# Scores of k's first 128 channels ahead of the others, and another order of M's pieces, in a fused attention and two-layer kernel

## The chip, the cores and the metric

The kernel runs on one core of a Trainium2 chip. The metric is the device time of one execution in microseconds; before the change it is 1213.12 us, the median of 3 runs (1212.65 to 1213.14).

## The reference

Shapes: q, k, v are 1 x 6016 x 256, w_in is 256 x 2048, w_out 2048 x 256, w_gate and w_val 256 x 1536, the last w_out 1536 x 256, all float32.

```python
qn = q / (norm(q, axis=1) + 1e-6);  kn = k / (norm(k, axis=1) + 1e-6)
s = kn.transpose(0, 2, 1) @ qn / tau          # 256 x 256, contracted over 6016 tokens
a = exp(s - s.max(-1));  a /= a.sum(-1) + 1e-9
x = v @ a                                     # 6016 x 256
h = x @ w_in                                  # 6016 x 2048
g = (a0 + a1 h + a2 h^2 + a3 h^3) / (1 + |b0||h| + |b1| h^2 + 1e-6)
y = g @ w_out                                 # 6016 x 256
out = (sigmoid(y @ w_gate) * (y @ w_val)) @ w_out2
```

The kernel computes M = a @ w_in once (256 x 2048), so that h = v @ M.

## The kernel before, in words

Each engine has a program of its own, written out by hand; between engines there are only semaphores, and each engine works its queue in order. Nothing plans or reorders. SP's queue (and ScalarE's for the first small chunks) issues the loads.

**Scores.** k and q arrive as 47 tiles of 128 tokens in 16 chunks (sizes 1 1 1 1 2 2 3, then 4). For each tile TensorE (L840 to L847) multiplies k's channels 0 to 127 by q (c = 0) and k's channels 128 to 255 by q (c = 1), 256 columns each in full float32, which the trace shows as two records a product. The two sums stay in two PSUM banks. ScalarE squares each chunk (L421, L425), VectorE adds the squares (L620, L627). `norms()` (L820) sums them over the partitions with TensorE, at tile NORMS_AT = 42 of 47. ScalarE takes roots (L434 to L440), VectorE reciprocals (L632, L634).

**Softmax.** For c = 0 and 1 VectorE scales the scores (L637) and takes the row minimum of the negated ones (L639), ScalarE takes the exponential with its row sum (L446), TensorE turns it (L854, 2 transposes), VectorE copies it to SBUF as `att_t` (L642). TensorE runs 8 spare products (L850, no result is used) before the first turn.

**M in pieces.** `M_TILES` lists pieces (half c, columns lo to hi) of M. `m_tile` (L806) makes one with two products into one of four banks; `split_m` splits it into a high part (ScalarE, L412) and a low part (VectorE, L594), which also applies the row's 1/sum. The first M_FIRST = 4 pieces are made behind the turns; the others (`M_AT`) in slots 0 to 5 of block 0.

**Blocks.** The 6016 tokens go in 16 blocks of 376 columns. A block has 8 slots j, each with a pair of 128 channels of h: TensorE `hidden` (12 products in a three-product float32r scheme, L801 to L803), ScalarE reads h twice (in block 0 L496 and L498, later L532 and L535; the second raises `h_read`), `vb` (L506, L551), VectorE the rational function (L714, L716, `first_quad` L679, L685, L688, L695 in block 0; L745 to L777 later), TensorE adds w_out times g. In block 0 that uses the raw w_out (`add_raw_y`, L902) two slots behind. y's gate and value tiles follow a block behind, from slot 2 of block 1 on. From block 2 on a loop runs.

**Weights.** The 13 chunks of w_out, w_gate, w_val, w_out2 are staged raw, copied to a high part by ScalarE (`weights_hi`, L400) and a low part by GpSimd (`weights_lo`, L372, from two SBUF operands). A chunk's staging space is reused by a later chunk, whose load on SP's queue waits for the low part. Before: high parts 0 to 3 before the norms, 4 after them, 5 behind M's first pieces, 6 to 12 in slots 1 to 7 of block 0; low parts 0 to 4 before the blocks, 5 in slot 0, 6 to 11 in slots 2 to 7, 12 in slot 0 of block 1, each after `h_read`. TensorE waits for all low parts in slot 2 of block 1 (L952).

Of the kernel before, what the change touches and what calls it, by code (L numbers as in the profile page):

```python
# [20 lines left out]
def attention_rational_gated_kernel(nc, q, k, v, tau, w_in, w_out1, coef_a, coef_b, w_gate, w_val, w_out2, out):  # L21
# [34 lines left out]
    M_BOUNDS = [0, P, 2 * P, 4 * P] + list(range(6 * P, FF1, BANK)) + [FF1]  # L56
    M_TILES = [(c, lo, hi) for lo, hi in zip(M_BOUNDS, M_BOUNDS[1:]) for c in range(CC)]
    M_FIRST = 4
    M_LOW = sum(lo < FF1 // 2 for _, lo, _ in M_TILES)
    M_AT = ((4, 5, 6, 7), (8, 9), (10,), (11,), (12,), (13,))  # L60
    assert M_FIRST + sum(len(a) for a in M_AT) == len(M_TILES)
# [9 lines left out]
    assert sum(KQ_SIZES) == NT  # L71


    W1_CHUNKS = T1 // 4
    EARLY_HI, EARLY_LO, COEF_AFTER = 6, 5, 6
    COEF_SPREAD_BEFORE = 9
    FIRST_SPARES, SOFTMAX_SPARES, SEAM_SPARES = 5, 8, 7
    NORMS_AT = NT - 5

    with ExitStack() as ctx:  # L80
# [96 lines left out]
        ps_attt = [ps[:, 6 + c, 0:C].rearrange("p (a b) -> p a b", a=CC) for c in range(CC)]  # L177
# [7 lines left out]
        kq_multiplied, squared, summed = sem("kq_multiplied"), sem("squared"), sem("summed")  # L185
        norms_summed, norms_rooted, small_step = sem("norms_summed"), sem("norms_rooted"), sem("small_step")
# [42 lines left out]
        assert EARLY_HI + PAIRS - 1 == EARLY_LO + PAIRS == len(chunks)  # L229
# [122 lines left out]
        def _(pool):  # L352
# [26 lines left out]
            def step(i, first, carry, head, tail):  # L379
                for j, now, late, old, gone, early, second, left in slots(i, first, carry, head, tail):  # L380
                    if is_block(i, 0) and j != 1 or is_block(i, 1) and j == 0:
                        pool.wait_ge(h_read, now + 1)
                        weights_lo(EARLY_LO + max(now - 1, 0))
                    if old is not None and not unsplit(old):
                        n = j % 2
                        pool.wait_ge(g_hi_ready, old + 1)
                        wait_count(pool, y_added, old + (-1))
                        nc.gpsimd.tensor_tensor(g_lo[n], g[n], as_f32(g_hi[n]),  # L388
                                                ALU.subtract).then_inc(g_lo_ready, 1)
# [5 lines left out]
        def _(act):  # L395
# [12 lines left out]
            def split_m(n):  # L408

                c, lo, hi = M_TILES[n]  # L410
                act.wait_ge(m_done, n + 1)
                nc.scalar.activation(m_hi[:, c, lo:hi], ps[:, M_BANKS[n % len(M_BANKS)], 0:hi - lo], ACT.Identity,  # L412
                                     scale=row_inv[:, c:c + 1]).then_inc(m_hi_ready, 1)
# [16 lines left out]
            act.wait_ge(kq_multiplied, sum(2 * t * C < 2 * CC * FF1 + 2 * T1 * C for t, _ in KQ_CHUNKS))  # L430
            for n in range(W1_CHUNKS):
                weights_hi(n)
# [10 lines left out]
            weights_hi(W1_CHUNKS)  # L443
# [4 lines left out]
            act.wait_ge(exps_ready, CC)  # L448
            nc.scalar.activation(row_sum, row_sum, ACT.Identity, bias=sum_guard).then_inc(sums_guarded, 1)
            act.wait_ge(row_inv_ready, 1)  # L450
            for n in range(M_FIRST):
                split_m(n)
            weights_hi(W1_CHUNKS + 1)
# [30 lines left out]
            def first_slot(j):  # L484
# [25 lines left out]
                if j != 1:  # L510
                    first_seed(max(j - 1, 0))
                if j > 0:
                    weights_hi(EARLY_HI + j - 1)

            def step(i, first, carry, head, tail):
                if splits_v(i, first):
                    split_v(i)
                for j, now, late, old, gone, early, second, left in slots(i, first, carry, head, tail):
# [26 lines left out]
                    if is_block(i, 1) and j == 1:  # L545
                        act.wait_ge(w_lo_ready, len(chunks))
# [38 lines left out]
        def _(dve):  # L585
# [49 lines left out]
            dve.wait_ge(kq_multiplied, len(KQ_CHUNKS))  # L635
            for c in range(CC):
                link(nc.vector.scalar_tensor_tensor(out=att[:, c, :], in0=ps_kq[:, c, :], scalar=k_inv[:, c:c + 1],  # L637
                                                    in1=q_inv, op0=ALU.mult, op1=ALU.mult))
                nc.vector.tensor_reduce(neg_min[:, c:c + 1], att[:, c, :], AX_X, ALU.min).then_inc(scores_ready, 1)  # L639
            for c in range(CC):  # L640
                dve.wait_ge(att_turned, c + 1)
                nc.vector.tensor_copy(att_t[:, :, c * P:(c + 1) * P], ps_attt[c]).then_inc(att_t_ready, 1)  # L642
            dve.wait_ge(sums_guarded, 1)
            nc.vector.reciprocal(row_inv, row_sum).then_inc(row_inv_ready, 1)
            dve.wait_ge(row_inv_ready, 1)
# [151 lines left out]
        def _(pe):  # L797
# [35 lines left out]
            spare_products(FIRST_SPARES)  # L833
            for n, (t, w) in enumerate(KQ_CHUNKS):
# [5 lines left out]
                for x in range(w):  # L840
                    if t + x == NORMS_AT:
                        norms()
                    for c in range(CC):
                        last = nc.tensor.matmul(ps_kq[:, c, :], k_in[n][:, x * C + c * P:x * C + (c + 1) * P],  # L844
                                                q_in[n][:, x * C:(x + 1) * C],
                                                start=(t + x == 0), stop=(t + x == NT - 1))
                last.then_inc(kq_multiplied, 1)  # L847

            pe.wait_ge(ident_ready, 1)
            spare_products(SOFTMAX_SPARES)  # L850
            for c in range(CC):
                pe.wait_ge(exps_ready, c + 1)
                for d in range(CC):
                    last = nc.tensor.transpose(ps_attt[c][:, d, :], att_e[:, c, d * P:(d + 1) * P], ident[:])  # L854
                last.then_inc(att_turned, 1)
            for n in range(M_FIRST):
                m_tile(n)

            def hidden(i, j, pair):
# [8 lines left out]
                for x in range(2):  # L868
                    f = slice((2 * j + x) * P, (2 * j + x + 1) * P)
                    if is_block(i, 0):  # L870
                        pe.wait_ge(m_lo_ready, sum(lo < f.stop for _, lo, _ in M_TILES))
# [126 lines left out]
```

## Time and profile before

| | |
|---|---|
| median of 3 runs | 1213.12 us |
| the profiled execution | 1212.42 us |
| its span | 1210.0 us |
| TensorE busy | 1195.0 us (99%) |
| VectorE busy | 1068.1 us (88%) |
| ScalarE busy | 882.5 us (73%) |
| GpSimd busy | 250.4 us (21%) |
| granted TensorE clock | 1.00 |

The span is what the profiler saw from the first to the last instruction; the execution's own time is somewhat longer. Busy TensorE is modelled: its products are pipelined and a row's length reaches over the next one's start, so the distance between starts is what one costs. A timeline row with a count is several instructions put together, from the first one's start to the last one's end. "idle before" is what an engine stood for in front of a row, and the arrow says who released it. In the chain of waits pieces follow each other without overlap. PE is TensorE, PEld its weight loads, DVE VectorE, ACT ScalarE, POOL GpSimd; `work`, `ps` and `before` are big buffers which hold many things.

### The profile page before, as it was taken

The page shows a single profiled execution, that of the slowest core. Times are in us where ns is not written, and L with a number is a line of the kernel's source. Part 1 is how long each engine was busy: PE and PEld are TensorE (multiplying, and loading weights), DVE is VectorE, ACT ScalarE, POOL GpSimd, SP SyncE. Part 2 cuts the span into 40 slices and gives each one's busy share as a digit, 9 for nine tenths or more (in the row PEclk, how much of TensorE's full clock was granted, in tenths as well). Part 3 has the DMA queues.
Part 4 walks back from the last instruction along what each step waited for, and adds up shares of the span by engine and source line. Part 5 has one row for each costly group of instructions (what it writes and reads, how often), then busy time and mean ns, then how long its engine had stood idle before and what let it go on. Part 6 is the DMA issues. An engine that isn't in the chain of part 4 may idle for free.

```text
span 1210.0 us, 19588 instructions
## 1 busy us (share of the span) xinstructions
PE 1195.0 (99%) x6804; PEld 1170.5 (97%) x6804; DVE 1068.1 (88%) x1373; ACT 882.5 (73%) x1267; POOL 250.4 (21%) x147
## 2 busy tenths in 40 slices
PE   9998999999999999999999999999999999999998
PEld 8866999999999999999999999999999999999998
DVE  7799999899998989998998999999899999989843
ACT  6897777677777767777786776778677777868632
POOL 0432212122212212211221221212112121212110
PEclk9999999999999999999999999999999999999999
DMA  9820000000000000000000000000000000000000
GB/s 361 303 65 13 1 14 14 13 0 13 13 13 13 13 13 0 13 13 13 13 13 13 13 0 13 13 13 13 13 13 0 13 13 13 13 0 13 0 14 14
DMA packets 15867, 33.83 MB, mean 28 GB/s; under 512 B 1382, under 2 KB 6246, under 8 KB 15846
## 3 DMA queue, kind: packets, MB, share of 16 engines
q1 hardware_dynamic: 14982, 32.51, 7.6%
q10 hardware_dynamic: 864, 1.05, 0.3%
q8 instruction: 12, 0.20, 0.1%
q14 instruction: 9, 0.07, 0.0%
HBM read 27.39 MB, written 6.16 MB: 28 GB/s over the span
## 4 chain that ended last, share of the span: by engine, by line
PE 92%; DVE 5%; issue 1%; ACT 1%; POOL 0%; DVEq 0%; ACTq 0%; POOLq 0%
PE ps L803 17%; PE ps L801 17%; PE ps L802 17%; PE ps L888 7%; PE ps L889 7%; PE ps L890 7%; PE ps L924 5%; PE ps L926 5%; PE ps L925 5%; PE ps L844 4%; PE ps L902 1%; DVE work L777 1%; DVE work L759 0%; DVE work L657 0%; DVE ys L674 0%
## 5 line engine op out<-in xcount | busy, mean ns | idle before, releaser
L388 POOL TENSOR_TENSOR g_parts<-work,g_parts 128x752 fp32r<-128x752 f32 x120 | 218.7, 1822 | 829.4 <-ACT g_parts L542 829.4
L532 ACT ACTIVATE work<-ps,neg_a 128x752 f32<-128x752 f32 x120 | 117.6, 980 | 145.2 <-PE ps L803 84.2
L801 PE MATMUL ps<-v_hi,m_hi 128*128 128x376 f32 x512 | 172.8, 338 | 0.6 <-DVE v_lo L588 0.3
L803 PE MATMUL ps<-v_hi,m_lo 128*128 128x376 f32 x512 | 171.5, 335 | 0.0
L802 PE MATMUL ps<-v_lo,m_hi 128*128 128x376 f32 x512 | 170.5, 333 | 0.0
L888 PE MATMUL ps<-g_parts,w_hi 128*128 128x376 f32 x480 | 160.6, 334 | 0.0
L889 PE MATMUL ps<-g_parts,w_hi 128*128 128x376 f32 x480 | 160.0, 333 | 0.0
L890 PE MATMUL ps<-g_parts,w_lo 128*128 128x376 f32 x480 | 159.4, 332 | 0.0
L652 DVE TENSOR_TENSOR work<-work,ps 128x376 f32<-128x376 f32 x192 | 103.8, 541 | 52.3 <-PE ps L803 39.3
L759 DVE TENSOR_TENSOR work<-work,ps 128x752 f32<-128x752 f32 x120 | 112.1, 934 | 38.1 <-ACT work L535 36.5
L568 ACT ACTIVATE work<-work,consts 128x752 f32<-128x752 int32 x120 | 110.2, 919 | 41.2 <-DVE work L777 41.2
L801 PE MATMUL ps<-ys,wg_hi 128*128 128x376 f32 x384 | 128.0, 333 | 3.6 <-ACT work L458 2.8
L463 ACT ACTIVATE ys<-work 128x376 fp32r<-128x376 f32 x192 | 98.6, 514 | 45.0 <-PE ps L926 44.8
L924 PE MATMUL ps<-ys,w_hi 128*128 128x376 f32 x384 | 129.2, 336 | 0.2 <-DVE ys L674 0.2
L803 PE MATMUL ps<-ys,wv_lo 128*128 128x376 f32 x384 | 128.7, 335 | 0.0
L474 ACT ACTIVATE work<-work,consts 128x752 f32<-128x752 f32 x120 | 110.7, 923 | 24.7 <-DVE work L745 24.7
L803 PE MATMUL ps<-ys,wg_lo 128*128 128x376 f32 x384 | 128.5, 335 | 0.0
L926 PE MATMUL ps<-ys,w_lo 128*128 128x376 f32 x384 | 128.5, 335 | 0.0
L802 PE MATMUL ps<-ys,wg_hi 128*128 128x376 f32 x384 | 127.9, 333 | 0.0
L925 PE MATMUL ps<-ys,w_hi 128*128 128x376 f32 x384 | 127.9, 333 | 0.0
L802 PE MATMUL ps<-ys,wv_hi 128*128 128x376 f32 x384 | 127.9, 333 | 0.0
L801 PE MATMUL ps<-ys,wv_hi 128*128 128x376 f32 x384 | 127.6, 332 | 0.0
(123 smaller groups left out, 2868.5 us busy)
## 6 DMA issues: line engine op xcount, KB each, us to landing
work<-in_v SPq DMA_DIRECT2D x16, 376.0 KB, 3.1
out<-work SPq DMA_DIRECT2D x15, 376.0 KB, 2.3
kq<-in_k SPq DMA_DIRECT2D x9, 512.0 KB, 13.7
kq<-in_q SPq DMA_DIRECT2D x9, 512.0 KB, 15.1
before<-in_moe_w_out SPq DMA_DIRECT2D x5, 512.0 KB, 12.6
before<-in_moe_w_in SPq DMA_DIRECT2D x8, 256.0 KB, 8.2
before<-in_moe_w_gate SPq DMA_DIRECT2D x2, 512.0 KB, 9.7
before<-in_moe_w_val SPq DMA_DIRECT2D x2, 512.0 KB, 6.8
```

The source lines that it names most:

```text
L388: nc.gpsimd.tensor_tensor(g_lo[n], g[n], as_f32(g_hi[n]), ALU.subtract).then_inc(g_lo_ready, 1)
L532: nc.scalar.activation(poly[n], ps_h, ACT.Identity, scale=neg_a[:, 3:4], bias=neg_a[:, 2:3])
L759: nc.vector.tensor_tensor(poly[n], poly[n], ps_h, ALU.mult).then_inc(horner1, 1)
L801: nc.tensor.matmul(dst, l_hi, r_hi, start=(n == 0), stop=False)
L802: nc.tensor.matmul(dst, l_hi, r_lo, start=False, stop=False)
L803: last = nc.tensor.matmul(dst, l_lo, r_hi, start=False, stop=(n == len(parts) - 1))
L888: nc.tensor.matmul(acc_y[:, c, :], l_hi, r_hi, start=(j == 0 and x == 0), stop=False)
L889: nc.tensor.matmul(acc_y[:, c, :], l_hi, r_lo, start=False, stop=False)
L890: last = nc.tensor.matmul(acc_y[:, c, :], l_lo, r_hi, start=False, stop=(j == PAIRS - 1 and x == 1))
L924: nc.tensor.matmul(acc_o[:, c, :], l_hi, s_hi[n], start=(m == 0), stop=False)
L925: nc.tensor.matmul(acc_o[:, c, :], l_hi, s_lo[n], start=False, stop=False)
L926: last = nc.tensor.matmul(acc_o[:, c, :], l_lo, s_hi[n], start=False, stop=(m == T2 - 1))
```

## The change

1. All products of half c = 0 run as tiles arrive; those of c = 1 trail behind, so that when the last chunk is done for c = 0, 29 of 47 are done for c = 1. KQ_LATE counts, before each chunk, how many c = 1 products are behind the program: 0 1 1 2 3 4 6 9 11 14 16 19 21 24 26 29.
2. The 18 products of c = 1 that are left follow, with `norms()` in front of number 38 and the turn of the first half in front of number 45. The 8 spares go.
3. VectorE and ScalarE take each half through the whole softmax, reciprocal of the row sum included, before the other; ScalarE's high part 3 stands between the two halves.
4. M's pieces: 12 in place of 14. Two of c = 0, 256 columns each, stand behind the scores and before the second turn; two of c = 1, 128 each, behind it. Slot 0 of block 0 has 256, 512 and 256 columns (before four times 256), slot 1 has 512 (before twice 512), slots 2 and 3 have 512 as before, slot 4 has 512 (before 256), slot 5 has 256.
5. Weights: high parts 0 and 1 before the norms (after the 32nd product of c = 1), 2 after them, 3 between the halves, 4 behind M's first pieces, 5 and 6 in slot 1 of block 0, 7 to 12 in slots 2 to 7. Low parts 0 to 3 before the blocks, 4 in slot 0, 5 to 10 in slots 2 to 7, 11 and 12 in slots 0 and 1 of block 1.

```diff
@@ -53,12 +53,17 @@
-    M_BOUNDS = [0, P, 2 * P, 4 * P] + list(range(6 * P, FF1, BANK)) + [FF1]
-    M_TILES = [(c, lo, hi) for lo, hi in zip(M_BOUNDS, M_BOUNDS[1:]) for c in range(CC)]
-    M_FIRST = 4
-    M_LOW = sum(lo < FF1 // 2 for _, lo, _ in M_TILES)
-    M_AT = ((4, 5, 6, 7), (8, 9), (10,), (11,), (12,), (13,))
-    assert M_FIRST + sum(len(a) for a in M_AT) == len(M_TILES)
+    M_TILES = [(0, 0, 256), (0, 256, 512), (1, 0, 128), (1, 128, 256), (1, 256, 512), (0, 512, 1024), (1, 512, 768),
+               (1, 768, 1280), (0, 1024, 1536), (1, 1280, 1792), (0, 1536, 2048), (1, 1792, 2048)]
+    M_BEHIND_SCORES, M_FIRST = 2, 4
+    M_AT = ((4, 5, 6), (7,), (8,), (9,), (10,), (11,))
+    assert M_FIRST + sum(len(a) for a in M_AT) == len(M_TILES) and CC == 2 and FF1 == 2048
+
+    def m_tiles_for(lo, hi):
+
+        return 1 + max(n for n, (_, m_lo_at, m_hi_at) in enumerate(M_TILES) if m_lo_at < hi and lo < m_hi_at)
+
+    M_LOW = m_tiles_for(0, FF1 // 2)

...
@@ -69,13 +74,14 @@
+    KQ_LATE = [0] + [min(t + w, 31 * (t + w + nxt) // 50) for (t, w), nxt in zip(KQ_CHUNKS, KQ_SIZES[1:] + [0])]
-    EARLY_HI, EARLY_LO, COEF_AFTER = 6, 5, 6
+    EARLY_HI, EARLY_LO, COEF_AFTER = 5, 4, 6
-    FIRST_SPARES, SOFTMAX_SPARES, SEAM_SPARES = 5, 8, 7
-    NORMS_AT = NT - 5
+    FIRST_SPARES, SEAM_SPARES = 5, 7
+    NORMS_AT, TURN_AT = NT - 9, NT - 2

...
@@ -378,7 +385,7 @@
-                    if is_block(i, 0) and j != 1 or is_block(i, 1) and j == 0:
+                    if is_block(i, 0) and j != 1 or is_block(i, 1) and j < 2:

...
@@ -409,6 +416,7 @@
+                act.wait_ge(row_inv_ready, c + 1)

...
@@ -427,8 +435,8 @@
-            act.wait_ge(kq_multiplied, sum(2 * t * C < 2 * CC * FF1 + 2 * T1 * C for t, _ in KQ_CHUNKS))
-            for n in range(W1_CHUNKS):
+            act.wait_ge(kq_multiplied, -(-(2 * CC * FF1 + 2 * T1 * C) // (2 * C)))
+            for n in range(2):

...
@@ -440,17 +448,20 @@
-            weights_hi(W1_CHUNKS)
+            weights_hi(2)
-            act.wait_ge(exps_ready, CC)
-            nc.scalar.activation(row_sum, row_sum, ACT.Identity, bias=sum_guard).then_inc(sums_guarded, 1)
-            act.wait_ge(row_inv_ready, 1)
+                act.wait_ge(exps_ready, c + 1)
+                nc.scalar.activation(row_sum[:, c:c + 1], row_sum[:, c:c + 1], ACT.Identity,
+                                     bias=sum_guard).then_inc(sums_guarded, 1)
+                if c == 0:
+                    weights_hi(3)
-            weights_hi(W1_CHUNKS + 1)
+            act.wait_ge(kq_multiplied, NT)
+            weights_hi(W1_CHUNKS)

...
@@ -509,8 +520,10 @@
+                if j == 1:
+                    weights_hi(EARLY_HI)
-                    weights_hi(EARLY_HI + j - 1)
+                    weights_hi(EARLY_HI + j)

...
@@ -542,7 +555,7 @@
-                    if is_block(i, 1) and j == 1:
+                    if is_block(i, 1) and j == 2:

...
@@ -632,17 +645,19 @@
-            dve.wait_ge(kq_multiplied, len(KQ_CHUNKS))
+                if c == 0:
+                    dve.wait_ge(first_scores, 1)
+                else:
+                    dve.wait_ge(kq_multiplied, NT)
-            for c in range(CC):
-            dve.wait_ge(sums_guarded, 1)
-            nc.vector.reciprocal(row_inv, row_sum).then_inc(row_inv_ready, 1)
-            dve.wait_ge(row_inv_ready, 1)
+                dve.wait_ge(sums_guarded, c + 1)
+                nc.vector.reciprocal(row_inv[:, c:c + 1], row_sum[:, c:c + 1]).then_inc(row_inv_ready, 1)
+            dve.wait_ge(row_inv_ready, CC)

...
@@ -831,6 +846,19 @@
+            def score(t, c):
+
+                n = max(n for n, (first, _) in enumerate(KQ_CHUNKS) if first <= t)
+                x = t - KQ_CHUNKS[n][0]
+                return nc.tensor.matmul(ps_kq[:, c, :], k_in[n][:, x * C + c * P:x * C + (c + 1) * P],
+                                        q_in[n][:, x * C:(x + 1) * C], start=(t == 0), stop=(t == NT - 1))
+
+            def turn(c):
+                pe.wait_ge(exps_ready, c + 1)
+                for d in range(CC):
+                    last = nc.tensor.transpose(ps_attt[c][:, d, :], att_e[:, c, d * P:(d + 1) * P], ident[:])
+                last.then_inc(att_turned, 1)
+

...
@@ -838,22 +866,22 @@
-                    if t + x == NORMS_AT:
-                        norms()
-                    for c in range(CC):
-                        last = nc.tensor.matmul(ps_kq[:, c, :], k_in[n][:, x * C + c * P:x * C + (c + 1) * P],
-                                                q_in[n][:, x * C:(x + 1) * C],
-                                                start=(t + x == 0), stop=(t + x == NT - 1))
-                last.then_inc(kq_multiplied, 1)
-
+                    last = score(t + x, 0)
+                if n == len(KQ_CHUNKS) - 1:
+                    last.then_inc(first_scores, 1)
+                for late in range(KQ_LATE[n], KQ_LATE[n + 1]):
+                    score(late, 1).then_inc(kq_multiplied, 1)
-            spare_products(SOFTMAX_SPARES)
-            for c in range(CC):
-                pe.wait_ge(exps_ready, c + 1)
-                for d in range(CC):
-                    last = nc.tensor.transpose(ps_attt[c][:, d, :], att_e[:, c, d * P:(d + 1) * P], ident[:])
-                last.then_inc(att_turned, 1)
-            for n in range(M_FIRST):
+            for late in range(KQ_LATE[-1], NT):
+                if late == NORMS_AT:
+                    norms()
+                if late == TURN_AT:
+                    turn(0)
+                score(late, 1).then_inc(kq_multiplied, 1)
+            for n in range(M_BEHIND_SCORES):
+                m_tile(n)
+            turn(1)
+            for n in range(M_BEHIND_SCORES, M_FIRST):

...
@@ -868,7 +896,7 @@
-                        pe.wait_ge(m_lo_ready, sum(lo < f.stop for _, lo, _ in M_TILES))
+                        pe.wait_ge(m_lo_ready, m_tiles_for(f.start, f.stop))

```

## Rows read from the trace of the kernel before

**Rows 1.** TensorE's timeline: start us, us, engine, line, operation, out<-in, count [idle before]

```profile
22.61 20.12 PE L844 MATMUL ps<-kq 128*128 128x256 f32 x92
...
49.67 0.44 PE L854 MATMUL ps<-ident,work 128*128 128x128 f32 x2
...
50.52 0.44 PE L854 MATMUL ps<-ident,work 128*128 128x128 f32 x2 [0.41 <-ACT work L446]
...
55.26 3.61 PE L815 MATMUL ps<-before 128*128 128x256 f32 x16
```

**Rows 2.** The chain of waits, 40 to 130 us: start us, us, engine and line

```profile
43.61 4.33 PE ps L844 x20
...
51.48 1.60 PE ps L815 x12
...
66.84 0.66 DVE m_lo L594
```

**Rows 3.** A window (us, PEld busy, clock, DMA share, GB/s); a wait, 53 to 125

```profile
47.90:53.10 5.20, 3.94 (x36) 1.00 1.00 365
...
PE ps L902 <- DVE work L695: 5.8, 6, 1.8
```

**Rows 4.** VectorE's timeline, 38 to 110 us

```profile
38.79 1.96 DVE L627 TENSOR_TENSOR work<-work 128x512 f32<-128x512 f32 x4
...
44.61 1.75 DVE L632 RECIPROCAL work<-work 128x256 f32<-128x256 f32 x1 [3.00 <-ACT work L437]
...
48.05 0.48 DVE L637 SCALAR_TENSOR_TENSOR work<-ps,small,work 128x256 f32<-128x256 f32 x1 [1.49 <-PE ps L844]
...
58.59 1.16 DVE L679 TENSOR_TENSOR work<-work 128x752 f32<-128x752 f32 x1
...
75.00 0.94 DVE L714 TENSOR_TENSOR work<-work,ps 128x752 f32<-128x752 f32 x1 [0.43 <-ACT work L498]
```

**Rows 5.** ScalarE's timeline, to 110 us

```profile
11.79 0.84 ACT L421 ACTIVATE work<-kq 128x768 f32<-128x768 f32 x1 [0.39 <-DMA kq<-in_q]
...
49.02 0.51 ACT L446 ACTIVATE work<-work,small 128x256 f32<-128x256 f32 x1 [1.80 <-DVE small L639]
...
57.18 0.47 ACT L412 ACTIVATE m_hi<-ps,small 128x256 fp32r<-128x256 f32 x1 [0.33 <-PE ps L815]
...
64.49 0.69 ACT L412 ACTIVATE m_hi<-ps,small 128x512 fp32r<-128x512 f32 x1
...
65.06 1.07 ACT L400 ACTIVATE wg_hi<-before 128x1024 fp32r<-128x1024 f32 x1
66.46 0.98 ACT L496 ACTIVATE work<-ps,neg_a 128x752 f32<-128x752 f32 x1 [0.34 <-PE ps L803]
```

**Rows 6.** Timelines where GpSimd and VectorE meet: block 0, block 1's start, the end

```profile
56.57 2.38 POOL L372 TENSOR_TENSOR wv_lo<-before,wv_hi 128x1024 fp32r<-128x1024 f32 x1 [3.26 <-ACT work L492]
...
108.03 2.38 POOL L372 TENSOR_TENSOR w_lo<-work,w_hi 128x1024 fp32r<-128x1024 f32 x1 [4.99 <-ACT work L535]
...
109.87 1.33 DVE L777 TENSOR_TENSOR work<-work 128x752 f32<-128x752 f32 x1
...
113.68 0.78 ACT L535 ACTIVATE work<-ps 128x752 f32<-128x752 f32 x1
...
113.94 0.93 DVE L745 SCALAR_TENSOR_TENSOR work<-work 128x752 f32<-128x752 f32 x1
...
114.79 1.00 DVE L749 SCALAR_TENSOR_TENSOR work<-work,neg_a 128x752 f32<-128x752 f32 x1
...
117.72 0.44 PE L801 MATMUL ps<-v_hi,m_hi 128*128 128x376 f32 x1 [0.18 <-DVE work L765]
...
1152.34 0.94 DVE L657 SCALAR_TENSOR_TENSOR work<-work 128x752 f32<-128x752 f32 x1
...
1152.82 2.14 POOL L388 TENSOR_TENSOR g_parts<-work,g_parts 128x752 fp32r<-128x752 f32 x1 [8.93 <-ACT g_parts L542]
...
1153.38 2.37 DVE L664 SCALAR_TENSOR_TENSOR work<-work 128x752 f32<-128x752 f32 x1
```

More of the change, by code:

```diff
@@ L176, in attention_rational_gated_kernel @@
         M_BANKS = (2, 3, 6, 7)
-        ps_attt = [ps[:, 6 + c, 0:C].rearrange("p (a b) -> p a b", a=CC) for c in range(CC)]
+        ps_attt = [ps[:, 4 + c, 0:C].rearrange("p (a b) -> p a b", a=CC) for c in range(CC)]
         coef_in, coef_spread = sem("coef_in"), sem("coef_spread")
@@ L185, in attention_rational_gated_kernel @@
         kq_multiplied, squared, summed = sem("kq_multiplied"), sem("squared"), sem("summed")
+        first_scores = sem("first_scores")
         norms_summed, norms_rooted, small_step = sem("norms_summed"), sem("norms_rooted"), sem("small_step")
@@ L228, in attention_rational_gated_kernel @@
             chunks.append((w2_v[:, 4 * n:4 * n + 4, :], w2_hi[:, 4 * n:4 * n + 4, :], w2_lo[:, 4 * n:4 * n + 4, :]))
-        assert EARLY_HI + PAIRS - 1 == EARLY_LO + PAIRS == len(chunks)
+        assert EARLY_HI + PAIRS == EARLY_LO + PAIRS + 1 == len(chunks)
         def staged(n):
```

## The prediction

> **What bounds the kernel now.** I read the chain of waits first, over the stretch before the steady loop. From the start to 47.9 us it is TensorE on the score products, 188 records for 94 products, at 20.12 / 46 = 0.437 us a product [rows 1]; the sums of squares are turned into norms inside that stream, between 22.61 + 20.12 = 42.73 and 43.61 [rows 1, 2]. From 47.9 to 53.1 the chain goes hand to hand: VectorE scales the scores, ScalarE takes the exponential, TensorE turns it, VectorE copies, TensorE makes M's first pieces (51.48 to 53.08 [rows 2]). The 36 weight loads there include the 8 spares [rows 3], which compute nothing. From 53.1 to about 120 us (block 0 and the seam to block 1) VectorE and ScalarE hold the chain: TensorE's product with the raw w_out1 waited on VectorE's L695 for 5.8 us in 6 times, 1.8 the longest [rows 3]. Thereafter TensorE is the bound and nothing absorbs a delay: what the stages up to 120 us gain or lose is what the end gains or loses. So every step is told as a shift against the old time at the same instruction.
>
> **1. The score stream.** All 94 products stay; only their order changes: first half of each tile, second half trailing. Before, the norms stood behind 84 products (42 tiles); now NORMS_AT = 38 puts them behind 47 + 38 = 85, which is +0.44. VectorE has the sums ready at 38.79 + 1.96 = 40.75 [rows 4], so that wait isn't the last. The other cost is data: the first half runs ahead of the old order. The tightest place is the chunk of 3 tiles: ScalarE waited for it until 11.79 [rows 5]. TensorE ended product 38 at about 22.37 (before the coefficient product ahead of 22.61 [rows 1]), so it reaches this chunk, now behind 14 products and not 16, at 22.37 - 24 x 0.437 = 11.88. Bounds 0 and 0.3; I take 0.06, for the margin is a tenth of a microsecond. The margins after it grow (the last chunk is reached behind 72 products, near 37.4). Norms: +0.5.
>
> **2. First half: norms to first turn.** The reciprocal L632 [rows 4] and what leads to it follow the norms and shift by 0.5. The old scaling L637 started at 48.05 after an idle 1.49 in which it waited for TensorE [rows 4]; that wait goes, so it starts at 48.05 - 1.49 + 0.5 = 47.06. From L637 to the exponential is 49.02 - 48.05 = 0.97 [rows 4, 5], from there to the turn 49.67 - 49.02 = 0.65 [rows 1, 5]. The turn can go at 47.06 + 0.97 + 0.65 = 48.68. TensorE gets there sooner: norms end at 43.61 + 0.5 = 44.11, and 7 of the 9 products left, at 4.33 / 10 = 0.433 [rows 2], end at 47.14. It **stands for 1.5 us before the turn**, with two score products and everything behind them in its queue. This is the wait that the change adds.
>
> **3. Second half.** The turn holds TensorE between 0 and 0.44, its row's length [rows 1]; I take 0.25, about the middle, since rows reach over the next start. The two products end at 48.68 + 0.25 + 0.87 = 49.80, where before all were done at 43.61 + 4.33 = 47.94 [rows 2]. Then 0.11 to the scaling, 0.97, 0.65: second turn at 51.53, and TensorE's two wide pieces (4 products of 256 columns by 0.437 = 1.75) end at 51.55. The old second turn started at 50.52 [rows 1]: **+1.03**. The old spares are no loss. Behind the second turn the piece with the second half's first 128 channels is again the first, so the old distance from 50.52 to hidden(0) at about 53.1 stays (bound: one 128 piece less, 1.60 / 3 = 0.53 better [rows 2]; I take none, since hidden waits for this piece's two splits, which don't shorten). hidden(0): +1.03.
>
> **4. Slot 0 of block 0.** Tile 5 is now 512 columns where it was 256. TensorE's two products take 2 x 0.437 longer = 0.87 (old pieces from 55.26 [rows 1]); its ScalarE split takes 0.69 for 0.47 [rows 5], 0.22 more; and that split stands ahead of vb, on which the chain hung (0.33 idle for TensorE at 57.18 [rows 5]). Against that, L679 took 1.16 at 58.59 [rows 4] because GpSimd ran until 56.57 + 2.38 = 58.95 [rows 6]; now it comes after GpSimd: -0.23. Sum +0.86, shift 1.9.
>
> **5. Slots 1 to 7.** Slot 1 has one 512 piece less: VectorE's split on the chain (66.84, 0.66 [rows 2]) goes, and ScalarE's 0.59 (64.49 to about 65.06 [rows 5]). But ScalarE gets a second weight chunk there (L400, 1.07, about 0.97 by starts [rows 5]); it had 0.34 idle before slot 2's L496 [rows 5]. So ScalarE's next reads come at 1.9 - 0.59 + 0.97 - 0.34 = +1.94, and VectorE's slot 2 at about +1.85. In slot 3 VectorE was idle for 0.43 [rows 4]: shift 1.4. Slot 4's piece grows by 256 columns (TensorE 0.87, VectorE 0.27); TensorE's waits on L695 [rows 3] cover it, if that is gone it costs 0.3. One w2 chunk's load is issued a slot later, as are v's next load behind it on SP's queue; both have slots of (109.87 - 58.59) / 8 = 6.4 us in hand [rows 4, 6]. **Shift into block 1: +1.4.**
>
> **6. The last low weight part, moved into slot 1 of block 1.** GpSimd's low parts start when ScalarE has read h. Here that is L535, 113.68 + 0.78 = 114.46 [rows 6]. VectorE then is in L745 (two operands from SBUF), and L749 (again two) follows at once at 114.79 [rows 6]. What the trace shows of such a meeting: GpSimd's L388 was issued at 1152.82 inside L657, ended at 1154.96, and VectorE's L664, issued at 1153.38, lasted 2.37 where it lasts 0.94: it ended 0.79 behind GpSimd. L777 at 109.87 in the same way ended (111.20) 0.8 behind the low part from 108.03 [rows 6]. By that, GpSimd waits for L745, runs 114.85 to 117.23, and L749 starts there and not at 114.79: **+2.4**. TensorE's next hidden already waits for VectorE there (0.18 at 117.72 [rows 6]), so it moves with it. Bounds: 0, if VectorE's queued L749 is let in first (then GpSimd falls beside operations that read PSUM), and 2.4. I take 2.3: the nearest row is that of 1152.82, where the waiting GpSimd went in first, less its gap of 0.1. The wait of TensorE for all low parts (low part done at 117.2; TensorE there at 117.72 + 12 products, about 119.7) isn't the last.
>
> The Trainium skill (SBUF — State Buffer, on the shared port pair) says that a VectorE operation with two SBUF inputs and a GpSimd one that reads SBUF exclude each other for a whole instruction, and the first to issue wins. By that rule GpSimd, issued at 114.5, goes before L749. It speaks against this change; by it the sum is the one taken here. The rows agree, except that none has two VectorE operations without a gap.
>
> **Sum.** 0.5 (1) + 0.53 (2, 3) + 0.86 - 0.49 (4, 5) + 2.3 (6) = +3.7. The profiled execution took 1212.42 us (span 1210.0, 2.4 around it), 0.7 below the median 1213.12. So 1216.1 by its time, 1216.8 by the median. What a measurement can tell from no change I take as 0.2%, 2.4 us: from 1210.7 to 1215.5.
>
> **Rivals.**
> A. VectorE goes first at step 6. For it: L749 stands in VectorE's queue with no gap, the row at 1152.82 had one of 0.1. Cost 0: +1.4, 1214.5, not slower by the bound. The point from which it decides: whether GpSimd's operation starts its 2.4 us before or after L749. Chance 0.33.
> B. The stall of step 2 doesn't come, and the second half runs as if hidden: scores end at 47.14 + 0.25 + 0.87 = 48.26, second turn at 50.0, hidden(0) 0.5 sooner than before; with steps 4 and 5 (+0.37) and A's outcome the time is 1213.0. It needs the first exponential 1.5 us earlier than the durations in [rows 4, 5] give. Chance 0.08; a third of it below 1210.7.
> C. TensorE's clock. With 8 spares gone it stands for 1.5 us and again in pieces up to hidden(0). The granted clock was 1.00 (2.4 GHz) in 47.9 to 53.1 [rows 3], and later waits of up to 1.8 us [rows 3] did not lower it; against C. If it fell to 1.2 GHz at 49 us, the second turn's pieces, hidden(0) and the slot's pieces (0.5 + 2 + 2.6 us of TensorE on the chain) would double, up to +5: near 1220. The Trainium skill (TensorE: Matmul & The Clock Gate, part 1) says that idleness brings the half rate back; on 1.8 us the trace disagrees. Chance 0.07.
> Something unnamed: 0.10.
>
> **How the numbers follow.** The forecast has 0.42, with a range of its own of 1216.0 to 1217.8. Slower by over 0.2%: 0.41 + 0.05 of A + 0.07 + 0.03 = 0.56. Within: 0.28 of A + 0.05 of B + 0.04 = 0.37. Faster: 0.07. The range reaches over A with its unknown 0.3 to 0.5 us to each side: 1213.4 to 1218.4.
>
> **What would show it.** Step 1: norms near 43.2 to 44.1. Step 2: an idle of 1.5 us of TensorE before the first turn at 48.7. Step 3: second turn at 51.5, hidden(0) at 54.1. Step 4: ScalarE's split of tile 5 near 59.0. Step 5: block 1's first hidden 1.4 later than before. Step 6: a 2.4 us L372 in block 1's slot 1 and an L749 of 3.4 us. I am wrong if TensorE doesn't wait at the first turn, or if L749 keeps its 1.0.

## The result, and the profile after

The changed kernel takes 1217.30 us (median of 8 executions, 1215.14 to 1219.09) against 1212.88 (8, 1211.42 to 1213.44) on the same chip: ratio 1.0036, 95% interval 1.0025 to 1.0047. It is slower, clear of the noise. The forecast was +3.7 us and 1216.8. The lowest times are 3.7 apart, the medians 4.4, and the profiled executions 1217.06 and 1212.42: 4.6 (spans 1215.1 and 1210.0: 5.1). That the distance differs with the way it is taken is the second half of this story: TensorE's clock falls for a few us in some executions and not in others.

The lines after the change are 7 to 28 higher than before; the prediction's lines are now: L637 is L653, L594 L607, L412 L420, L372 L379, L679 L694, L695 L710, L745 L760, L749 L764, L765 L780, L777 L792, L801 L816, L815 L830, L844 L853, L854 L859, L902 L930.

TensorE's timeline of the kernel after, up to the first hidden product (start us, us, engine, line, operation, out<-in, count, idle before and what ended it); it answers to [rows 1, 2]:

```profile
3.77 4.66 PE L853 MATMUL ps<-kq 128*128 128x256 f32 x14
8.71 11.82 PE L853 MATMUL ps<-kq 128*128 128x256 f32 x52 [0.28 <-DMA kq<-in_q]
...
43.69 0.68 PE L840 MATMUL ps<-work,ones 128*128 128x256 f32 x2
44.20 3.18 PE L853 MATMUL ps<-kq 128*128 128x256 f32 x14
48.98 0.44 PE L859 MATMUL ps<-ident,work 128*128 128x128 f32 x2 [1.59 <-ACT work L454]
49.25 1.03 PE L853 MATMUL ps<-kq 128*128 128x256 f32 x4
50.12 1.89 PE L830 MATMUL ps<-before 128*128 128x256 f32 x8
51.95 0.44 PE L859 MATMUL ps<-ident,work 128*128 128x128 f32 x2
52.90 1.16 PE L830 MATMUL ps<-before 128*128 128x128 f32 x8 [0.52 <-DVE before L657]
54.55 0.41 PE L816 MATMUL ps<-v_hi,m_hi 128*128 128x376 f32 x1 [0.49 <-DVE m_lo L607]
```

hidden(0) is the first hidden product of block 0. The first turn waits 1.59 us for ScalarE's exponential, with the last scores behind it; the second turn is at 51.95 where it was at 50.52 (+1.43), and hidden(0) at 54.55 where it was at 53.12 (+1.43).

VectorE's timeline after, slots 0 and 1 of block 0 and slot 1 of block 1; it answers to [rows 4, 6]:

```profile
61.07 0.94 DVE L694 TENSOR_TENSOR work<-work 128x752 f32<-128x752 f32 x1
...
69.03 0.94 DVE L710 SCALAR_TENSOR_TENSOR work<-work 128x752 f32<-128x752 f32 x1
...
117.18 0.94 DVE L760 SCALAR_TENSOR_TENSOR work<-work 128x752 f32<-128x752 f32 x1
118.03 3.10 DVE L764 SCALAR_TENSOR_TENSOR work<-work,neg_a 128x752 f32<-128x752 f32 x1
121.05 0.93 DVE L774 TENSOR_TENSOR work<-work,ps 128x752 f32<-128x752 f32 x1
```

GpSimd's timeline after, the moved low part:

```profile
117.78 2.55 POOL L379 TENSOR_TENSOR w_lo<-work,w_hi 128x1024 fp32r<-128x1024 f32 x1 [4.14 <-ACT work L548]
```

GpSimd's operation was issued while L760 ran and ended at 120.33. L764, which stands behind L760 without a gap, was held until then and ended at 121.13, 0.80 later. Ahead of it the shift was 117.18 - 113.94 = 3.24; the next operation's is 121.05 - 115.70 = 5.35. That is +2.11 for one moved operation. Of the 5.35, 0.17 go in a later wait of TensorE's (129.51 for 124.34); the rest reaches the end, where the span grew by 5.1.

What the prediction does not have lies between, in slot 2 of block 0. Weight loads of TensorE (PEld), with the time that they stood; then the chain of waits (start us, us, engine and line); then windows (us, PEld busy, granted clock, DMA share, GB/s), all of the kernel after:

```profile
70.02 0.97 PEld L930 LDWEIGHTS ps<-work,before 128*128 128x128 f32 x4 [3.02 <-DVE work L710]
```

```profile
69.11 0.86 DVE work L710
70.02 4.49 PE ps L930 x8
```

```profile
68.00:70.00 2.00, 0.00 (x0) 1.00 0.00 0
70.00:72.00 2.00, 1.16 (x6) 0.72 0.00 0
72.00:74.00 2.00, 1.13 (x4) 0.50 0.00 0
74.00:76.00 2.00, 1.77 (x11) 0.93 0.00 0
```

Slot 2's eight products with the raw w_out1 start at 70.02, and the weight loads stood for 3.02 us ahead of them. They take 4.49 us; before they took 2.79, started at 68.41 and had 1.10 of standing ahead of them. At half the rate (1.2 GHz) the granted clock stood for 2 x 0.28 / 0.5 + 2.0 + 2 x 0.07 / 0.5 = 3.4 us of these windows, and half of that is lost: 1.70 us of the shift are TensorE's clock, the same as 4.49 - 2.79. Put together along the span: 1.43 + 0.15 (slots 0 to 7, the pieces) + 1.70 (clock) gives 3.28 at block 1's first hidden (103.89 before, 107.17 after), and 2.11 more at L764.

Stands are counted here and below in the rows of the weight loads. Those of one of M's pieces are done before its products are, so in front of slot 2 this count is 0.82 longer than that of the products. The products' rows, of the kernel after and then of the kernel before:

```profile
70.02 4.49 PE L930 MATMUL ps<-work,before 128*128 128x376 f32 x8 [2.20 <-DVE work L710]
...
123.06 0.44 PE L816 MATMUL ps<-v_hi,m_hi 128*128 128x376 f32 x1 [2.28 <-DVE work L780]
```

```profile
124.34 0.44 PE L801 MATMUL ps<-ys,wg_hi 128*128 128x376 f32 x1 [2.24 <-ACT work L458]
```

Behind the first of the three the clock fell, behind the other two it stayed at 1.00, though they are no shorter. So the length of the stand alone does not decide.

Whole executions carry the same mark. Those of the kernel after with a mean clock of 1.0 took 1215.1 and 1215.4; those with 0.997 took 1218.7 and 1219.1. The kernel before has it too: of the 33 executions that stood beside four of the experiments, the 14 with a clock of 1.0 took 1211.3 to 1212.4, the 12 with 0.998 took 1212.6 to 1213.8. The seven with 0.999 took 1211.9 to 1213.6, on both steps: the mean clock is a blurred mark, since it also holds what comes behind the last product, where a fall costs nothing (0.82 in 1208 to 1210 of the kernel before, with no product left). A median of either kernel says how often its executions had a fall.

### The profile page after: what moved, and what is told of

The parts are those of the page before. It is cut to its first block, busy times and chain, and to the rows that moved or that the text cites. A ratio compares the mean times of both kernels' runs of the same rounds, so it can differ in the third digit from the quotient of the medians.

```text
span 1215.1 us, 19547 instructions
## 1 busy us (share of the span) xinstructions
PE 1194.6 (98%) x6780; PEld 1167.6 (96%) x6780; DVE 1069.8 (88%) x1372; ACT 881.5 (73%) x1266; POOL 250.7 (21%) x147
## 4 chain that ended last, share of the span: by engine, by line
PE 91%; DVE 5%; issue 1%; ACT 1%; DMA 1%; ACTq 0%; DVEq 0%
PE ps L818 17%; PE ps L816 17%; PE ps L817 17%; PE ps L916 7%; PE ps L917 7%; PE ps L918 7%; PE ps L952 5%; PE ps L954 5%; PE ps L953 5%; PE ps L853 3%; PE ps L930 1%; DMA kq<-in_q 1%; DVE work L764 1%; DVE work L792 1%; DVE work L774 0%
## 5 line engine op out<-in xcount | busy, mean ns | idle before, releaser
L816 PE MATMUL ps<-v_hi,m_hi 128*128 128x376 f32 x512 | 173.5, 339 | 2.9 <-DVE work L780 2.3
L816 PE MATMUL ps<-ys,wg_hi 128*128 128x376 f32 x384 | 128.2, 334 | 3.5 <-ACT work L469 2.6
L816 PE MATMUL ps<-ys,wv_hi 128*128 128x376 f32 x384 | 127.7, 333 | 0.0
```

Of the source, the lines that this page charges most:

```text
L816: nc.tensor.matmul(dst, l_hi, r_hi, start=(n == 0), stop=False)
```

## The experiments

Eleven kernels in three groups, each with the kernel before beside it on the same chip: the first four (e1 to e4) against 1212.85 (21 executions), the next four (e5, e6, b1, b2) against 1212.70 (33), the last three (e7, b3, b4) against 1211.63 (27). The three chips differ, and so does the share of executions with a fall; kernels of different groups are compared by their distance from the kernel before at a mean clock of 1.0 (medians 1211.69 in the second group, 1211.56 in the third, 14 executions each). Kernels e are the kernel after with an edit, kernels b the kernel before with one. Times are medians, with the lowest where it says more.

**The low part behind L764.** In GpSimd's program, before the low part of slot 1 of block 1:

```
+ if is_block(i, 1) and j == 1:
+     pool.wait_ge(scaled, PAIRS + 1)
  weights_lo(EARLY_LO + max(now - 1, 0))
```

> The changed kernel with one wait more: GpSimd's last low part (slot 1 of block 1) waits until VectorE's L764 is done. Port theory (GpSimd and a VectorE operation with two SBUF operands exclude each other; the one that waited first goes first): L764 is back from 3.10 to 1.00 us, the low part starts some 1.4 us later beside operations that read PSUM, and everything behind is 2.1 us earlier: 1215.2 against 1217.3 in the median. Rival (the low part's 2.4 us are on the chain themselves, TensorE's wait for all low parts in slot 2): the time stays at 1217.3 or grows, with a TensorE wait on GpSimd in slot 2. In both, TensorE's clock still falls in some executions in slots 1 and 2 of block 0, 1.7 us each time.

Its VectorE timeline, and GpSimd's:

```profile
118.04 1.00 DVE L766 SCALAR_TENSOR_TENSOR work<-work,neg_a 128x752 f32<-128x752 f32 x1
118.95 0.93 DVE L776 TENSOR_TENSOR work<-work,ps 128x752 f32<-128x752 f32 x1
```

```profile
119.17 2.37 POOL L379 TENSOR_TENSOR w_lo<-work,w_hi 128x1024 fp32r<-128x1024 f32 x1 [5.51 <-DVE work L766]
```

L764 (here L766) is back at 1.00 and what follows comes at 118.95, 2.10 sooner: step 6's mechanism and size are shown. Yet the kernel took 1216.82 (5 executions), 0.5 less than the kernel after and 1.6 more than expected. The rival's cause is not there either: no product from 100 to 140 us waits for GpSimd. The windows of the one execution that was traced show where the gain went:

```profile
68.00:72.00 4.00, 1.32 (x6) 0.88 0.00 0
72.00:76.00 4.00, 2.84 (x14) 0.70 0.00 0
...
120.00:128.00 8.00, 5.08 (x32) 1.00 0.00 1
128.00:132.00 4.00, 4.00 (x17) 0.63 0.00 0
132.00:136.00 4.00, 4.00 (x23) 0.94 0.01 2
```

The fall at 70 is there again, and a second one at 128, behind a wait of 2.55 us; the kernel after has none there in its profile. 4 us at 0.63 and 4 at 0.94 are 4 x 0.37 + 4 x 0.06 = 1.7 us of TensorE lost, on a stretch where TensorE is the bound. Its executions have clocks of 0.997 (four) and 0.998.

**TensorE kept at work in slot 2 of block 0.** Eight spare products before the product with the raw w_out1:

```
+ if is_block(i, 0) and j == 2:
+     spare_products(8, ps[:, 3, 0:P])
```

> The changed kernel with 8 spare products (1.8 us of TensorE, no result used) in slot 2 of block 0, behind M's piece, where TensorE stood for 3.0 us. Clock theory (the M piece of slot 1 that the change took away also kept TensorE's clock up): the clock stays at 1.00 in every execution, the product with the raw w_out1 takes 2.8 and not 4.5 us, the spans all lie near 1213.3, the median at 1215.5 with a spread under 1 us. Rival (the fall has another cause, the missing 8 spares of the softmax or chance): the clock still falls in about half of the executions, median 1217.3.

```profile
67.44 1.75 PEld L845 LDWEIGHTS ps<-ones 128*128 128x128 f32 x15 [0.24 <-issue]
69.80 2.19 PEld L930 LDWEIGHTS ps<-work,before 128*128 128x128 f32 x8 [0.60 <-DVE work L710]
```

The stand is 0.60 in place of 3.02, the clock is 1.00 from 60 to 124, and L764, still 3.10 long, starts at 116.21 and not at 118.03: 1.82 sooner, 0.23 of which were there at hidden(0) already. Median 1215.42 (8), 1.9 less than the kernel after. The products of ones compute nothing; the gain is the clock. Two parts of the expectation failed: the clock is not 1.00 in every execution (0.999 in seven of eight; the profiled one falls at 126 to 132, behind a stand of 2.38), and the spread is 1.6 us.

**M's pieces of before, in the order of after.** From tile 5 on the old widths (13 pieces; two in slot 1):

```
- M_AT = ((4, 5, 6), (7,), (8,), (9,), (10,), (11,))
+ M_AT = ((4, 5, 6), (7, 8), (9,), (10,), (11,), (12,))
```

> The changed kernel with M's pieces of before from tile 5 on: 256, 256, 256 columns in slot 0, twice 512 in slot 1, 512, 512, 256, 256 behind. By my steps: slot 0 gives back 0.87 + 0.22 us, less up to 0.3 because VectorE's first quad falls under GpSimd's low part again; slot 1 costs 0.66 more on VectorE; nothing for the piece sizes themselves, within 0.3 us. But TensorE is filled in slot 1, so the clock stays up: spans near 1213.3, median 1215.5. Rival (the piece sizes themselves are what the change pays for): 0.8 us or more below that.

Median 1215.42 (9), L764 at 116.47. The stand in slot 2 is 1.48 and the clock holds there; it falls at 120 to 126, behind a stand of 2.48. Against the kernel after L764 is 1.56 sooner; the clock gives 1.70 of it, and hidden(0) was 0.30 later here (54.85), so the old pieces are 0.16 sooner by their own durations, near the +0.15 of the result. Nearly all that the new ones cost is that they leave TensorE idle ahead of slot 2's raw product.

**Norms five products sooner.** `NORMS_AT = NT - 14` for `NT - 9`.

> The changed kernel with the norms in front of second-half product 33 and not 38, five products or 2.2 us earlier; the turn stays in front of number 45. Stall theory (the first turn waits for the chain from the norms): the norms' chain is earlier by about 1.5 us (ScalarE's high parts 0 and 1 end at 42.9 and hold its root back by 0.7), the stall of 1.6 us in front of the turn all but goes, hidden(0) starts near 53.1 to 53.2 and the time is 1.4 us less: 1215.9. Rival (M's first pieces or the low parts hold hidden(0), not the turn): the stall goes, but hidden(0) moves by under 0.5 us.

TensorE's timeline of this kernel:

```profile
42.05 5.34 PE L853 MATMUL ps<-kq 128*128 128x256 f32 x24
47.23 0.41 PE L859 MATMUL ps<-ident,work 128*128 128x128 f32 x2
...
52.78 0.41 PE L816 MATMUL ps<-v_hi,m_hi 128*128 128x376 f32 x1 [0.49 <-DVE m_lo L607]
```

The wait before the first turn is gone and hidden(0) comes at 52.78: 1.77 sooner than after. Some 0.4 of that is the start-up of this execution, in which no chunk was waited for: over all profiles hidden(0) stands at 53.21 in the mean with the norms here (e4 to e7) and at 54.56 where the change has them (after, e1 to e3), 1.35 apart, as forecast (1.4). Steps 2 and 3 stand: the loss was the stall, and the stall was a matter of where the norms stand. Median 1215.40 (10). The clock fell at 68 to 72 all the same (0.60), behind the same 3.02 us: the fall does not need the stall before the turn.

**The low part in the kernel before.** One part later, as the change does it, and nothing else: `EARLY_LO` 4 for 5, released in slots 0 and 1 of block 1, and the wait for all low parts one slot later with it.

> The kernel before with one part of the change alone: GpSimd's low parts one slot later (4 in slot 0, 5 to 10 in slots 2 to 7, 11 and 12 in slots 0 and 1 of block 1). Port theory: in slot 1 of block 1 L749 lasts 3.1 us and not 1.0, everything behind is 2.1 us late: lowest run 1213.5 against 1211.4 of before, median 1214.9 against 1212.9. Rival (the low part finds room beside operations that read PSUM, and the 2.1 us of the changed kernel belong to another of its parts): the time of before.

```profile
114.93 2.54 POOL L372 TENSOR_TENSOR w_lo<-work,w_hi 128x1024 fp32r<-128x1024 f32 x1 [4.14 <-ACT work L535]
```

```profile
115.17 3.09 DVE L749 SCALAR_TENSOR_TENSOR work<-work,neg_a 128x752 f32<-128x752 f32 x1
```

The same pair of rows in the other kernel. Lowest 1213.29 against 1211.27 (+2.0), median 1213.65 (+0.95, where 2.0 was expected), ratio 1.0011 (1.0002 to 1.0020). At a mean clock of 1.0 it is +1.96: 1213.65 (three executions) against 1211.69 (14). None of its 11 executions has a clock under 0.999 where 12 of the 33 of the kernel before have 0.998; that it had fewer falls is the likely reason for the smaller distance of the medians. In its profile the fall stands at 120 to 124 (0.62), behind a wait of 2.47.

**All three mends.** The kernel after with low part, pieces and norms of the experiments above.

> The changed kernel with three steps undone or mended together: the last low part behind L764, M's pieces from tile 5 on as before, norms in front of product 33. If the steps add up, executions without a fall of TensorE's clock are 2.1 + 1.8 us below the changed kernel's lowest, 1215.1: 1211.3, the level of before (1211.4). What is left of the change then gains nothing. If clock falls come as in the single ones, the median is 1 to 1.5 us above that. Rival (the steps hide each other): lowest above 1212.5.

Median 1213.28 (11), ratio 1.0005 (0.9996 to 1.0014); the lowest, the only one with a clock of 1.0, is 1211.34. In the profiled one the wait of 2.52 us at 124.81 is followed by 0.71 and 0.86 in 124 to 132. The steps add up: with them undone the lowest time is that of the kernel before, and the median lies one fall of the clock (1.7 us) and a bit above it.

**Low parts let go by VectorE's last quotient.** In the kernel before, two short meetings of the same kind cost 0.39 each: L777 at 109.87 [rows 6] and L588, in its timeline:

```profile
102.51 1.33 DVE L588 TENSOR_TENSOR v_lo<-work,v_hi 128x752 fp32r<-128x752 f32 x1
```

From slot 3 on the low part is let go when g is ready (`g_ready`), a moment at which VectorE goes on to operations that read PSUM:

```
- pool.wait_ge(h_read, now + 1)
+ if now > 2:
+     pool.wait_ge(g_ready, now - 1)
+ else:
+     pool.wait_ge(h_read, now + 1)
```

> The kernel before with GpSimd's low parts from slot 3 of block 0 on released by VectorE's last quotient (g_ready) and not by ScalarE's second read of h. Where VectorE then stands for 0.4 to 0.6 us, GpSimd starts that much sooner and is done before VectorE's next operation with two SBUF operands: v's low part in slot 7 and L777 in slot 0 of block 1 take 0.94 and not 1.33 us. Port theory: 0.8 us less, 1212.1 in the median, lowest run 1210.6. Rival (these two are not on the chain): no change, within 0.2 us.

```profile
101.75 0.94 DVE L591 TENSOR_TENSOR v_lo<-work,v_hi 128x752 fp32r<-128x752 f32 x1
...
108.69 0.93 DVE L780 TENSOR_TENSOR work<-work 128x752 f32<-128x752 f32 x1
```

They last 0.94 and 0.93. From hidden(0) to L749 (here L752) it is 113.22 - 52.44 = 60.78 us, before 114.79 - 53.12 = 61.67: 0.89 less, so the two meetings were on the chain. Median 1212.08 (11; before 1212.70), ratio 0.9996 (0.9987 to 1.0005): not to be told from no change by this interval, though the lowest, 1209.94, is 1.3 under that of before.

**Everything, with the clock held.** e5 with that release, 4 spares in slot 2 of block 0 and 8 spares in slot 2 of block 1, ahead of its second gate product:

```
+ if is_block(i, 1) and j == 2:
+     spare_products(8, ps_spare_m)
  gate_and_value(*second)
```

> As the one before, with the low parts released by the quotient from slot 3 on, and 4 spare products in slot 2 of block 0 and 8 in slot 2 of block 1, where TensorE stands for over 2 us and the clock fell in other executions. Port theory and clock theory together: 0.8 us less and fewer falls: lowest 1210.5, median 1210.8 to 1211.5, faster than before (1212.9). Rival (falls come wherever, by chance): spread of 1.7 us as before, median 1212.

Median 1211.04 (11, 1210.65 to 1211.91), ratio 0.9991 (0.9982 to 1.0000). All 11 executions have a clock of 1.0. The spread fell from 2.9 us (e5) to 1.3. Against the kernel before at the same clock it is 0.65 less, about what the release of the low parts is worth; the rest of the distance between the medians (1.66) is the clock.

**The same without the new score order**, that is the kernel before with the release and the 8 spares:

> The kernel before, nothing of the change, with the two things that the changed kernel's study gave: low parts released by the quotient from slot 3 on, and 8 spare products in slot 2 of block 1. If these and not the new order of the scores make e6_best fast: lowest 1210.0, median 1210.4 to 1211.2, the time of e6_best (1211.0) or below it. Rival (the new order of scores and softmax is worth something once its costs are mended): 0.5 us or more above e6_best.

Median 1210.82 (11, 1210.01 to 1211.53), ratio 0.9992 (0.9983 to 1.0001), clock 1.0 in all 11. Against the kernel before at a clock of 1.0 on its chip it is 0.74 less, e6 0.65 on its own: as fast as e6. The new order of the scores gains nothing that is left at the end, even mended.

**The change's own pieces, mended.** The kernel after with norms early, the release, the low part behind L764, 8 spares in each of the two slots:

> As e6_best, but with the changed kernel's own pieces of M and 8 spare products in slot 2 of block 0 in place of the second piece in slot 1. Clock theory: with the clock held up the two lists of pieces cost the same within 0.2 us: 1211.0, clock 1.00. Rival (the list itself is worse, by its 512-column piece in slot 0): 0.5 us or more above e6_best.

Median 1211.09 (11), ratio 0.9994 (0.9985 to 1.0003), clock 1.0 in all. Against the kernel before at a clock of 1.0 it is 0.47 less, e6 0.65. With the clock held, the two lists of pieces are within 0.2 us of each other, as expected.

**One piece less in slot 1 of the kernel before**, to see whether that alone brings the clock down:

```
- M_AT = ((4, 5, 6, 7), (8, 9), (10,), (11,), (12,), (13,))
+ M_AT = ((4, 5, 6, 7), (8,), (9,), (10,), (11,), (12,), (13,))
```

> The kernel before with one part of the change alone: one 512-column piece of M in slot 1 of block 0 and not two; pieces 9 to 13 each one slot later. Clock theory: VectorE's first quotient comes 0.66 us earlier, but TensorE stands 1.1 us longer in front of the first product with the raw w_out1 (2.2 where it was 1.1), and its clock falls in slots 1 and 2 in the profiled execution and in most others: about 1.5 us each time, median 1213.3 to 1213.8, few runs under 1212. Rival (the falls of the changed kernel come from the spares taken away before the first turn, which are here): the clock stays at 1.00 there and the time is 1212.2 in the median, up to 0.6 less than before.

```profile
67.83 2.19 PEld L902 LDWEIGHTS ps<-work,before 128*128 128x128 f32 x8 [2.12 <-DVE work L695]
...
124.04 0.19 PEld L801 LDWEIGHTS ps<-ys,wg_hi 128*128 128x128 f32 x1 [2.55 <-ACT work L458]
```

Median 1211.44 (11), ratio 0.9997 (0.9988 to 1.0006): a miss for the expectation that the clock falls there. The stand there grew from 1.10 to 2.12, not to the 3.02 of the kernel after, and the clock stayed 1.00. In 4 of the 11 executions it is 0.998 or 0.999 (1212.5 to 1213.0), and in the profiled one of them the fall is at 124 to 128 (0.62), behind the wait of 2.55 that the kernel before has too. So a piece less in slot 1 is not enough by itself. At a clock of 1.0 this kernel is faster than the one before, 1211.16 (7) against 1211.56 (14), which is what its rival had. From here to the kernel after, TensorE's piece of slot 1 moves by 62.17 - 60.88 = 1.29, VectorE's first operation of the second slot (L685 at 61.68, L700 at 63.87) by 2.19; the 0.90 between them is what slot 0's wider split adds to ScalarE and VectorE behind TensorE's back (step 4), and it is the rest of the stand: 2.12 + 0.90 = 3.02 (by the products' rows 1.30 + 0.90 = 2.20). That sum is read from the rows; the wide tile alone was not run.

## Why the prediction was right, and where it was not

The sum was +3.7; where the clock holds, the kernel is slower by that (lowest against lowest, 1215.14 - 1211.42). That it agrees to a tenth is partly luck: the steps measured 1.43 + 0.15 + 2.11 = 3.69 where 1.03 + 0.37 + 2.3 = 3.70 was forecast, with errors of +0.40, -0.22 and -0.19 that cancel. The forecast time of 1216.8 is near the measured median for another reason too: its start, 1213.12, is a time that the kernel before takes with a fall of the clock (1211.3 to 1212.4 without one), so it holds one fall that no step of the sum names. By its steps:

1. Norms: +0.5 forecast, +0.75 measured (the second of the norms' products at 43.69, before at 42.94). The surplus is data: TensorE waited 0.28 us at 8.71 for a transfer of q, at an earlier chunk than the one that the prediction called the tightest. Over all profiles of the two orders this product stands at 42.25 to 43.38 (five with the order of before, mean 42.89) and at 43.46 to 43.99 (four with that of after, mean 43.70): +0.81. The waits for data at 6 to 10 us come and go in both, 0 to 1.1 us in sum, so one profile against another is good to half a microsecond in this stage.
2. The stall before the first turn: 1.5 forecast, 1.59 measured, first turn at 48.98 for 48.68. Right, and e4, where the stall and its cost go together, shows it.
3. Second turn and hidden(0): +1.03 forecast, +1.43 measured. 0.25 of the 0.40 comes from step 1; the turn and the two products behind it held TensorE for 50.12 - 48.98 = 1.14 where 1.12 was worked out. The rest is small gaps.
4. and 5. Slot 0 +0.86, slots 1 to 7 -0.49, together +0.37; measured 3.28 - 1.43 - 1.70 = +0.15. ScalarE's vb in slot 0 came at 60.04 for 57.55, a shift of 2.49 for 1.9 + 0.4 (the 0.4 from step 3); L679 became 0.94 from 1.16, as said. The sum is 0.22 too high. (One term in it, ScalarE's split of the dropped piece, was read as 0.59 where the starts give 65.06 - 64.49 = 0.57.)
6. The low part: 2.3 forecast, 2.11 measured. This is the step that decided against rival A, and it was carried by one row of the end of the trace [rows 6] where VectorE had a gap of 0.1; without a gap it goes the same way. By the Trainium skill (SBUF — State Buffer, on the shared port pair), the first to issue wins: GpSimd did, and the trace agrees in both kernels that have the meeting (3.10 and 3.09 us).

The rival that was priced wrongly is C, the clock. The prediction placed a fall before the first turn, where TensorE now stands for 1.59 us (1.99 in the rows of the weight loads), and found that later waits of up to 1.8 us did not lower it [rows 3]. That was right for that place: the clock stayed at 1.00 there. (The row has only the waits on L695; the longest wait of the same stretch was for ScalarE, 2.24 us at 124.34, and did not lower it in that profile either.) But the same change takes a piece out of slot 1 and delays VectorE in slot 0, and step 5 counted only VectorE's and ScalarE's splits of it. That TensorE's own 1.75 us of it would become standing ahead of slot 2's raw product was in no step. The stand there grew by 1.92 to 3.02 us, 1.02 of it by the missing piece (b3) and 0.90 by the delay, and the clock behind it fell, which cost 1.70. What the runs show is that the clock holds there when the stand is filled (e2, 0.60) or shortened (e3, 1.48); they give no rule that tells this stand from the one at 124.34, between products equally long (2.20 and 2.24), so it stays open why the clock fell behind the one and not behind the other. The measured median is above the forecast by this term; the lowest times are not. Rival B did not come; e4 shows what it would have needed.

Why the mended versions stop at a tenth of a per cent: norms early (1.35 between the means) and the low part behind L764 (2.10) only undo what the change added. With the stall gone, the new order brings the second turn, on which hidden(0) hangs, to 50.18, 50.25, 50.92 and 51.08 (e4, e6, e7, e5; mean 50.61); with the order of before it is at 49.84 to 50.96 (five profiles, mean 50.48). The first turn comes 2 us sooner, the second does not, since two products and a whole softmax of the second half stand between the two. The gain of e6 and b4 comes from GpSimd's release and from the clock.

## What to carry to other kernels

A piece of work taken out of a stretch where TensorE waits for others is not free there: it makes a stand longer, and a fall of the clock behind it may cost more than the piece saves. List TensorE's long stands before and after an edit, not only the chain, and say whether they are counted between products or between weight loads. Before moving a GpSimd operation that reads SBUF, look at what VectorE does when it is let go: let go just ahead of a two-operand read of SBUF it cost 2.1 of its 2.4 us here, beside reads of PSUM nothing that shows (e1, b2), and the semaphore that lets it go is a free choice. Compare executions of the same mean clock before explaining a difference of one part in a thousand, and take the mark for what it is: 0.999 can be either.

## What the runs showed of the hardware

After a stand of 3.02 us of the weight loads (2.20 of the products) the clock fell in all three profiles that have one (the kernel after, e1, e4), to 0.5 in the worst 2 us; two of the eight executions of the kernel after have a mean clock of 1.0, so it need not. After waits of 2.35 to 2.61 us (2.04 to 2.30 of the products) between 120 and 130 us it fell in six cases (e1, e2, e3, e5, b1, b3) and did not in seven (the kernel before; both of the kernel after; the first of e2; both of e4; b2). The kernel before and b3 have the same wait, 2.55, at 124.3 and 124.0, and it fell in one and not in the other. The waits of 1.0 to 2.12 us ahead of those products in block 0 were followed by none. What decides was not found; eight products that compute nothing there held the clock in all 33 executions of e6, e7 and b4. A fall takes 1.70 to 1.72 us from TensorE each time, in the windows of all nine falls that the profiles have before 136 us.

A waiting GpSimd operation goes in between two VectorE operations that follow each other without a gap: it does not need one. VectorE's held operation ends 0.80 us behind GpSimd's end, where it lasts 1.00 by itself: as if nearly all of its work came afterwards. GpSimd's own operation lasted 2.55 us for 2.37 where its start fell into the VectorE operation ahead; that the one lengthened the other is not shown by itself.
